# A chunked recurrence fused with two expert layers: the scores of both batch rows made where rows are turned, and their products in one run

## The chip, the cores and the metric

The kernel runs on one core of a Trainium2 chip. The metric is the device time of one execution in microseconds. The profile of the kernel before is one execution of it, with its own time.

## The reference, cut to what matters

Two batch rows of 768 positions, 8 heads of 48 columns. Three stages follow one another: a linear recurrence by heads, a dense layer pair with a normalization ahead of it, and a mixture of 8 experts in which each position goes to one.

```python
for t in range(S):                      # attention-like recurrence
    cur = np.einsum('bhd,bhe->bhde', u[None] * kt, vt)
    y[:, :, t] = np.einsum('bhd,bhde->bhe', rt, state + cur)
    state = w[None, :, :, None] * state + np.einsum('bhd,bhe->bhde', kt, vt)
x = y by position, 384 columns
xn = (x - mu) / np.sqrt(var + 1e-06) * g_ln
x = x + np.maximum(xn @ w_ch1, 0.0) @ w_ch2            # 384 -> 1536 -> 384
logits = x @ w_gate ; e = argmax, or the one before     # 8 experts, 384 -> 1024 -> 384
out[b, s] = p[e] * (np.maximum(x[b, s] @ w1[e], 0.0) @ w2[e])
```

## The kernel before

**Tiles.** The 1536 rows are 12 tiles of 128 positions, numbered c: tile c holds chunk c // 2 of batch row u = c % 2. Two tiles are a group, g = 0 to 5; I call g = 0 the first group, g = 1 the second, and so on. The recurrence is done by chunks. For each tile `scores` makes keys times queries inside the chunk (8 heads, two PSUM banks, halves of heads), VectorE multiplies them with a mask into `scT` (`masked`), `from_state` adds what the state carries in, `from_scores` what the masked scores give, both into one bank (this is the tile's product), and `gain` makes what the tile adds to the state. VectorE then does `new_state`, `sums` (product plus the diagonal part into `xs`) and `moments`; `rows_of` is the last two. The recurrence runs two tiles ahead of the dense layers: in group g the dense layers of tiles 2g, 2g + 1 are worked on, and the recurrence of tiles 2g + 2 and 2g + 3.

**The dense layers of a group.** `hidden(g, q)` makes pair q of six (q = 0 to 5): 18 matmuls of 256 columns into bank 6 or 7 by turns. ScalarE rectifies the pair into `hT_hi`, VectorE makes the remainder `hT_lo` (its `hidden`, line L1568) and counts `h_ready`. Two pairs later TensorE needs that bank again and waits for that count. `rows_out(g, u)` is the second layer, 36 matmuls into bank 5 - u; between its two calls `turn_xn(g + 1)` turns the normalized rows of the next group into banks 0 and 1. VectorE adds the result to the rows (`residual`), makes the turned rows' remainder (`turned`), and makes the gate columns of the expert layer (`gates`, L1677), nine for each tile, spread by hand between its other steps wherever nothing waits for them; a gate reads two tensors of SBUF, `x2` and `wgr`.

**What sets the order.** Every engine's program is written out by hand, with counting semaphores. In the kernel before, the loop body on TensorE is pairs 0 to 2, then `chunk` of the first tile (its gain and products), `scores` of the second tile, pairs 3 and 4, `chunk` of the second tile, pair 5, `rows_out`, `turn_xn`, `scores` of the next group's first tile in banks 2 and 3, and `rows_out`. GpSimd has a queue of its own order: `diagonal` of both tiles (after VectorE's `coefs`), then for each of the next two tiles `decays` (two products, L530 and L537, after the turned keys and queries of that tile have landed), `rows` (L548, L550) and `ends` (L563). SyncE's `load_turned(c)` waits until `from_state` of tile c - 2 is over, since it overwrites that tile's keys and queries.

```python
                for q in pairs:
                    if not isinstance(g, int) or g * NHP + q >= 2:
                        pe.wait_ge(h_ready, g * NHP + q - 1)
```

## Time and profile before

| what | us |
|---|---|
| median of 3 runs | 385.42 (384.82 to 387.62) |
| the profiled execution's own time | 384.97 |
| its span | 383.1 |
| mean granted TensorE clock | 0.996 |

The profiled execution took 1.9 us more than its span, and is 0.45 us below the median. The six groups fill the time from about 17 to 214 us of the span, the experts the rest.

### The profile page before, as it was taken

What the parts mean: (1) busy time and instruction counts of PE and PEld (TensorE: products, weight loads), DVE (VectorE), ACT (ScalarE), POOL (GpSimd) and SP (SyncE); (2) the same over time, 40 slices, a digit from 0 to 9 for tenths busy, and PEclk for the clock granted to TensorE, in tenths of its full rate; (3) what the DMA queues carried; (4) which work ended last, traced back from release to release, by engine and by line L of the source; (5) the groups of instructions that cost most, each with busy time, mean ns of one, the idle gap of its engine ahead of it and who ended that gap; (6) DMA issues with size and microseconds to landing.
All of it is one profiled execution on the core that took longest, in us unless ns stands there. A gap on an engine that the chain in (4) does not pass through costs nothing.

```text
span 383.1 us, 8871 instructions
## 1 busy us (share of the span) xinstructions
PE 372.5 (97%) x3056; PEld 338.6 (88%) x3056; DVE 285.5 (75%) x630; ACT 155.4 (41%) x281; POOL 137.5 (36%) x114
## 2 busy tenths in 40 slices
PE   8999999999999999999999999999999999999993
PEld 6899999999999999999999656789999999999982
DVE  7799899988897997868878568798546764647440
ACT  6556313212322221241441254368525852555530
POOL 2999784911760570100004006303332233223231
PEclk9999999999999999999999999999999999999998
DMA  7999603302500330500038484799874287111011
GB/s 218 328 329 285 212 22 113 112 21 67 157 36 21 110 110 26 181 3 22 21 97 286 134 308 144 264 372 305 301 277 151 87 277 284 43 34 43 26 45 43
DMA packets 32923, 56.67 MB, mean 148 GB/s; under 512 B 3294, under 2 KB 20484, under 8 KB 32753
## 3 DMA queue, kind: packets, MB, share of 16 engines
q1 hardware_dynamic: 30576, 49.84, 39.9%
q0 software_dynamic: 2304, 6.30, 5.3%
q8 instruction: 23, 0.38, 0.4%
q14 instruction: 20, 0.16, 0.1%
HBM read 51.41 MB, written 5.51 MB: 149 GB/s over the span
## 4 chain that ended last, share of the span: by engine, by line
PE 91%; DVE 5%; issue 1%; DMA 1%; ACT 1%; POOL 0%; SPq 0%; POOLq 0%; DVEq 0%; ACTq 0%
PE bank L1039 18%; PE bank L935 7%; PE bank L937 7%; PE bank L936 7%; PE bank L1367 5%; PE bank L1339 5%; PE bank L1375 5%; PE bank L1371 5%; PE bank L1343 5%; PE bank L1346 5%; PE bank L1356 3%; PE bank L953 3%; PE bank L1268 3%; PE bank L1245 3%; PE bank L984 2%; PE bank L974 2%
## 5 line engine op out<-in xcount | busy, mean ns | idle before, releaser
L1039 PE MATMUL bank<-xnT_hi,parts 128*128 128x256 f32 x432 | 65.3, 287 | 0.5 <-ACT xnT_hi L726 0.2
L1677 DVE SCALAR_TENSOR_TENSOR stage<-stage 128x384 f32<-128x384 f32 x81 | 60.7, 791 | 0.1
L1039 PEld LDWEIGHTS bank<-xnT_hi,parts 128*128 128x128 f32 x432 | 56.6, 191 | 2.0 <-ACT xnT_hi L726 0.5
L733 ACT ACTIVATE parts<-bank 128x512 fp32r<-128x512 f32 x36 | 21.5, 597 | 90.6 <-PE bank L1039 90.5
L667 POOL DMA_INDIRECT out_y<-late x14 | 20.5, 1462 | 93.9 <-DVE late L1964 93.9
L935 PE MATMUL bank<-parts 128*128 128x384 f32 x144 | 49.3, 342 | 0.0
L937 PE MATMUL bank<-parts 128*128 128x384 f32 x144 | 48.2, 335 | 0.0
L936 PE MATMUL bank<-parts 128*128 128x384 f32 x144 | 48.2, 334 | 0.0
L813 ACT ACTIVATE parts<-stage (+1 forms) x32 | 46.2, 1485 | 0.4 <-DMA stage<-in_w 0.4
L1933 DVE TENSOR_TENSOR parts<-stage,parts x24 | 41.1, 1755 | 4.9 <-ACT parts L813 4.2
L1039 PE MATMUL bank<-xnT_lo,parts 128*128 128x256 f32 x216 | 37.4, 282 | 0.0
L574 POOL TENSOR_TENSOR arena<-arena,coef 128x384 f32<-128x384 f32 x12 | 13.0, 1080 | 60.6 <-DVE coef L1458 60.3
L1568 DVE SCALAR_TENSOR_TENSOR parts<-bank,parts 128x512 fp32r<-128x512 f32 x36 | 24.8, 689 | 11.3 <-ACT parts L733 11.0
L1964 DVE TENSOR_SCALAR late<-bank,late 128x384 f32<-128x384 f32 x14 | 8.7, 618 | 32.9 <-PE bank L1375 32.6
L660 POOL DMA_INDIRECT late<-x_rows,late x18 | 22.3, 1241 | 28.2 <-DVE late L1890 23.0
L1039 PEld LDWEIGHTS bank<-xnT_lo,parts 128*128 128x128 f32 x216 | 30.9, 191 | 0.3 <-issue 0.3
L935 PEld LDWEIGHTS bank<-parts 128*128 128x128 f32 x144 | 27.1, 188 | 0.4
L936 PEld LDWEIGHTS bank<-parts 128*128 128x128 f32 x144 | 27.1, 188 | 0.0
L937 PEld LDWEIGHTS bank<-parts 128*128 128x128 f32 x144 | 27.0, 188 | 0.0
L1339 PE MATMUL bank<-parts,xnT_hi 128*128 (+1 forms) x84 | 26.6, 425 | 0.0
L904 ACT ACTIVATE heT_hi<-bank 128x512 fp32r<-128x512 f32 x28 | 15.2, 596 | 28.0 <-PE bank L1356 28.0
L1955 DVE TENSOR_TENSOR heT_lo<-bank,heT_hi 128x512 fp32r<-128x512 f32 x28 | 18.0, 683 | 11.0 <-ACT heT_hi L904 10.9
(257 smaller groups left out, 732.6 us busy)
## 6 DMA issues: line engine op xcount, KB each, us to landing
stage<-in_w SPq DMA_DIRECT2D x36, 768.0 KB, 6.7
stage<-in_w_ch SPq DMA_DIRECT2D x6, 768.0 KB, 7.8
arena<-in_k_t SPq DMA_DIRECT2D x12, 224.0 KB, 3.2
arena<-in_r_t SPq DMA_DIRECT2D x12, 224.0 KB, 3.1
arena<-in_v_rows SPq DMA_DIRECT2D x12, 192.0 KB, 3.9
arena<-in_k_rows SPq DMA_DIRECT2D x12, 192.0 KB, 3.2
x_rows<-stage SPq DMA_DIRECT2D x12, 192.0 KB, 1.9
arena<-in_r_rows SPq DMA_DIRECT2D x10, 192.0 KB, 3.3
```

The source lines that it names most:

```text
L660: pool.indirect_dma_start(xg[s % XR], None, x2_dram, bass.IndirectOffsetOnAxis(take[:, s:s + 1], 0)).then_inc(s_xg[s % XR], 16)
L667: pool.indirect_dma_start(out, bass.IndirectOffsetOnAxis(give[:, s:s + 1], 0), yo[s % 2], None, bounds_check=T - 1, oob_is_err=False).then ...
L733: act.activation(hT_hi[:, 2 * q:2 * q + 2, :].rearrange("p a t -> p (a t)"), bk[6 + q % 2][:], ACT.Relu).then_inc(h_hi_ready, 1)
L813: act.activation(e_at(b, 0, j), e_stage(h, j), ACT.Copy).then_inc(e_hi[j // EP], 1)
L935: pe.matmul(out_, a_lo, b_hi, start=start, stop=False)
L936: pe.matmul(out_, a_hi, b_lo, start=False, stop=False)
L937: return pe.matmul(out_, a_hi, b_hi, start=False, stop=stop)
L1039: mm = pe.matmul(acc, w[:, k, at], x[:, k, :], start=start and k == 0, stop=stop and k == KD - 1, skip_group_check=first and q == 0)
L1339: pe.matmul(bk[2 + half][:], xnT_hi[:, k, u], hi(k), start=k == 0, stop=False)
L1568: dve.scalar_tensor_tensor(hT_lo[:, at, :].rearrange("p a t -> p (a t)"), bk[6 + q % 2][:], 0.0, hT_hi[:, at, :].rearrange("p a t -> p (a ...
L1677: dve.scalar_tensor_tensor(spent[n % NSPENT], x2[t % 2], 1.0, wgr[e], ALU.mult, ALU.mult, accum_out=lg[:, t, e:e + 1]).then_inc(s_spent, 1)
L1933: dve.tensor_tensor(e_at(e & 1, 1, j), e_stage((e + 1) & 1, j), e_at(e & 1, 0, j).bitcast(F32), ALU.subtract).then_inc(e_lo[j // EP], 1)
```

## The change

**What it does.** From tile 4 on the scores of both tiles of the next group are made behind `turn_xn`, the first tile's in banks 6 and 7, the second's in banks 2 and 3. The masked scores of the two tiles go to two buffers, `scT[0]` and `scT[1]`. The products and gains of both tiles stand in one run behind pair 2, the first tile's in banks 4 and 3, the second's in banks 5 and 2. The second group makes its own scores behind its pair 0, in banks 0 to 3, and is now written out ahead of the loop, which runs over the third and the fourth group; the first group keeps its order, less the scores of tile 4 at its end. ScalarE scales both states (`decay`) in one place behind pair 1. VectorE masks the first tile's scores behind `turned`, makes both `coefs` behind pair 1, does both tiles' `new_state` and `rows_of` behind pair 2, and the gates are dealt out anew. SyncE's and GpSimd's programs are the same.

```diff
--- before.py
+++ after.py
@@ -753,13 +753,15 @@
                     round_piece(2)
                 hidden(g, range(1, 2))
                 decay(g * 2 + 2, 0)
+                if not first:
+                    decay(g * 2 + 3, 1)
                 hidden(g, range(2, 3))
...
-                decay(g * 2 + 3, 1)
+                    decay(3, 1)
@@ -940,11 +942,10 @@
                 if not isinstance(c, int) or c > 0:
                     pe.wait_ge(kdec_ready, c + 1)
                     pe.wait_ge(rdec_ready, c + 1)
-                if isinstance(c, int) and c < 4 and c >= 2 or u:
-                    if not isinstance(c, int) or c >= 2:
-                        pe.wait_ge(masked_ready, c * 2)
-                elif not isinstance(c, int) or c:
-                    pe.wait_ge(state_ready, c)
+                if isinstance(c, int) and 2 <= c <= 4:
+                    pe.wait_ge(masked_ready, c * 2)
+                elif u and not (isinstance(c, int) and c == 1):
+                    pe.wait_ge(state_ready, c - 1)
                 for p in range(NP_):
                     if isinstance(c, int) and c == 0:
                         pe.wait_ge(s_pair, p + 1)
@@ -1008,15 +1009,24 @@
                                        start=True, stop=True)
                 mm.then_inc(coef_mm, 1)
 
-            def chunk(c, u, n_lg, ends):
-                if ends:
-                    pe.wait_ge(state_ready, c)
-                    pe.wait_ge(masked_ready, c * 2 + 2)
-                    gain(c, u, bk[3])
-                if n_lg is not None:
-                    pe.wait_ge(x2_ready, n_lg)
-                from_state(c, u)
+            def first_chunk(c, u):
+                pe.wait_ge(state_ready, c)
+                gain(c, u, bk[3])
+                from_state(c, u, bk[4], c)
                 from_scores(c, u, bk[4], scT[0])
+
+            def chunks(g, ends):
+                c = g * 2 + 2
+                pe.wait_ge(masked_ready, c * 2 + 4)
+                pe.wait_ge(x2_ready, g * 2)
+                for u in range(2):
+                    if ends:
+                        pe.wait_ge(state_ready, c)
+                        gain(c + u, u, bk[3 - u])
+                    else:
+                        pe.wait_ge(s_rows[u], R_FIRST[u] + R_LOADS * (c // 2))
+                    from_state(c + u, u, bk[4 + u], c)
+                    from_scores(c + u, u, bk[4 + u], scT[u])
 
             def turn_xn(g):
                 for u in range(2):
@@ -1074,6 +1084,7 @@
             def rows_out(g, u, between=()):
                 if u == 0:
                     if not isinstance(g, int) or g >= 1:
+                        pe.wait_ge(x_ready, NT if isinstance(g, int) and g >= NG - 2 else g * 2 + 4)
                         pe.wait_ge(x2_ready, g * 2 - 1)
                 else:
                     pe.wait_ge(x_ready, NT if isinstance(g, int) and g >= NG - 2 else g * 2 + 4)
@@ -1125,32 +1136,34 @@
 
             def group(g, ends=True):
                 first = isinstance(g, int) and g == 0
-                n_lg = None if first else g * 2
 
                 pe.wait_ge(xnT_hi_ready, g * 2 + 2)
                 if first:
                     hidden(g, range(0, 2))
-                    scores(g * 2 + 2, 0, bk[0:2])
+                    scores(2, 0, bk[0:2])
                     hidden(g, range(2, 3))
-                    chunk(g * 2 + 2, 0, n_lg, ends)
+                    first_chunk(2, 0)
                     hidden(g, range(3, 5))
-                    scores(g * 2 + 3, 1, bk[0:2])
+                    scores(3, 1, bk[0:2])
                     hidden(g, range(5, NHP))
-                    chunk(g * 2 + 3, 1, n_lg, ends)
+                    first_chunk(3, 1)
                 else:
-                    hidden(g, range(0, 3))
-                    chunk(g * 2 + 2, 0, n_lg, ends)
-                    scores(g * 2 + 3, 1, bk[0:2])
-                    hidden(g, range(3, 5))
-                    chunk(g * 2 + 3, 1, n_lg, ends)
-                    hidden(g, range(5, NHP))
+                    if isinstance(g, int) and g == 1:
+                        hidden(g, range(0, 1))
+                        scores(4, 0, bk[0:2])
+                        scores(5, 1, bk[2:4])
+                        hidden(g, range(1, 3))
+                    else:
+                        pe.wait_ge(masked_ready, g * 4 + 6)
+                        hidden(g, range(0, 3))
+                    chunks(g, ends)
+                    hidden(g, range(3, NHP))
                 rows_out(g, 0)
                 turn_xn(g + 1)
                 if not first and ends:
-                    scores(g * 2 + 4, 0, bk[2:4])
+                    scores(g * 2 + 4, 0, bk[6:8])
+                    scores(g * 2 + 5, 1, bk[2:4])
                 rows_out(g, 1)
-                if first:
-                    scores(4, 0, bk[2:4])
 
             scores(0, 0, bk[0:2])
             pe.wait_ge(s_const, 16)
@@ -1175,7 +1188,8 @@
             keep_warm(1)
             group(0)
             pe.wait_ge(s_gw, 16)
-            with pe.Fori(1, NG - 2) as g:
+            group(1)
+            with pe.Fori(2, NG - 2) as g:
                 group(g)
             group(NG - 2, ends=False)
 
@@ -1461,8 +1475,8 @@
             def masked(c, banks, sc, halves=range(2)):
                 for half in halves:
                     dve.wait_ge(score_mm, c * 2 + half + 1)
-                    if not isinstance(c, int) or c >= 2:
-                        dve.wait_ge(y_mm, c)
+                    if c >= 2:
+                        dve.wait_ge(y_mm, c if c < 5 else c - 1)
                     dve.tensor_tensor(sc[:, NP_ * half:NP_ * (half + 1), :],
                                       banks[half][:].rearrange("p (a t) -> p a t", a=NP_),
                                       mask, ALU.mult).then_inc(masked_ready, 1)
@@ -1679,37 +1693,32 @@
 
             def group(g, ends=True):
                 t0, t1 = (g - 1) * 2, (g - 1) * 2 + 1
+                c0, c1 = g * 2 + 2, g * 2 + 3
                 if g > 1:
-                    gates(t0, range(4, 5))
+                    gates(t0, range(3, 5))
                 hidden(g, range(0, 1))
-                if not ends:
-                    coefs(g * 2 + 2, 0)
-                masked(g * 2 + 2, bk[2:4], scT[0])
-                gates(t0, range(5 if g > 1 else 4, 7))
+                if g == 1:
+                    masked(c0, bk[0:2], scT[0])
+                masked(c1, bk[2:4], scT[1])
+                if g > 1:
+                    gates(t0, range(5, 6))
                 hidden(g, range(1, 2))
-                if ends:
-                    coefs(g * 2 + 2, 0)
-                gates(t0, range(7, 8))
+                coefs(c0, 0)
+                coefs(c1, 1)
+                gates(t0, range(4 if g == 1 else 6, 7))
                 hidden(g, range(2, 3))
-                if ends:
-                    new_state(g * 2 + 2, 0, bk[3])
-                rows_of(g * 2 + 2, 0, bk[4])
-                if not ends:
-                    coefs(g * 2 + 3, 1)
-                masked(g * 2 + 3, bk[0:2], scT[0])
-                if ends:
-                    coefs(g * 2 + 3, 1)
-                gates(t0, range(8, E + 1))
+                for c, u in ((c0, 0), (c1, 1)):
+                    if ends:
+                        new_state(c, u, bk[3 - u])
+                    rows_of(c, u, bk[4 + u])
+                gates(t0, range(7, E + 1))
                 hidden(g, range(3, 4))
-                gates(t1, range(0, 1))
+                gates(t1, range(0, 2))
                 hidden(g, range(4, 5))
-                if ends:
-                    new_state(g * 2 + 3, 1, bk[3])
-                rows_of(g * 2 + 3, 1, bk[4])
                 means(g + 1)
-                gates(t1, range(1, 2))
+                gates(t1, range(2, 4))
                 hidden(g, range(5, NHP))
-                gates(t1, range(2, E + 1))
+                gates(t1, range(4, E + 1))
                 rows_done(g)
 
             def rows_done(g):
@@ -1718,8 +1727,10 @@
                     flags(0)
                 residual(g, 0)
                 turned(g + 1)
+                if 0 < g < NG - 2:
+                    masked(g * 2 + 4, bk[6:8], scT[0])
                 if g < NG - 2:
-                    gates(g * 2, range(0, 4))
+                    gates(g * 2, range(0, 3 if g else 4))
                 elif g == NG - 2:
                     gates(g * 2, range(0, 6))
                 residual(g, 1)
```

On TensorE, in the body of the loop before (second to fourth group), from the first tile's gain (L965) to pair 3; the REGISTER_ALU rows make the semaphores' targets:

```order
L965 MATMUL bank<-arena 48x48 x8
L970 REGISTER_ALU
L974 MATMUL bank<-arena 64x96 x8
L980 REGISTER_ALU
L984 MATMUL bank<-arena 64x48 x16
L941 REGISTER_ALU
L945 REGISTER_ALU
L953 MATMUL bank<-arena 128x128 x8
L1045 REGISTER_ALU
L1039 MATMUL bank<-xnT_hi,parts 128x256 x6
```

In the changed kernel the same place, in the second group, which is written out (the loop has the same order); L1049 is the pairs' matmul, L966 the gain, L975 and L985 the products:

```order
L1049 MATMUL bank<-xnT_lo,parts 128x256 x3
L966 MATMUL bank<-arena 48x48 x8
L975 MATMUL bank<-arena 64x96 x8
L985 MATMUL bank<-arena 64x48 x16
L966 MATMUL bank<-arena 48x48 x8
L975 MATMUL bank<-arena 64x96 x8
L985 MATMUL bank<-arena 64x48 x16
L1049 MATMUL bank<-xnT_hi,parts 128x256 x6
```

The second tile's gain and product now follow the first tile's at once, and the scores (L953 there) are gone from the place.

On VectorE, in the third group of the kernel before, from the gate ahead of pair 2 to pair 3 (L1677 gate, L1568 pair, L1481 and L1482 new state, L1488 and L1496 `rows_of`, L1466 masks, L1458 coefs):

```order
L1677 SCALAR_TENSOR_TENSOR stage,lg<-stage 128x384
L1568 SCALAR_TENSOR_TENSOR parts<-bank,parts 128x512
L1481 TENSOR_TENSOR arena<-bank,arena 48x4x48
L1482 TENSOR_TENSOR arena<-bank,arena 48x4x48
L1488 TENSOR_TENSOR stage<-bank,arena 128x384
L1496 BN_STATS stats<-stage 128x6
L1466 TENSOR_TENSOR arena<-bank,cst 128x512 x2
L1458 TENSOR_REDUCE coef<-arena 128x8
L1677 SCALAR_TENSOR_TENSOR stage,lg<-stage 128x384
L1568 SCALAR_TENSOR_TENSOR parts<-bank,parts 128x512
```

In the changed kernel, same group and same two pairs (L1691 gate, L1582 pair, L1495 and L1496 new state, L1502 and L1510 `rows_of`):

```order
L1691 SCALAR_TENSOR_TENSOR stage,lg<-stage 128x384
L1582 SCALAR_TENSOR_TENSOR parts<-bank,parts 128x512
L1495 TENSOR_TENSOR arena<-bank,arena 48x4x48
L1496 TENSOR_TENSOR arena<-bank,arena 48x4x48
L1502 TENSOR_TENSOR stage<-bank,arena 128x384
L1510 BN_STATS stats<-stage 128x6
L1495 TENSOR_TENSOR arena<-bank,arena 48x4x48
L1496 TENSOR_TENSOR arena<-bank,arena 48x4x48
L1502 TENSOR_TENSOR stage<-bank,arena 128x384
L1510 BN_STATS stats<-stage 128x6
L1691 SCALAR_TENSOR_TENSOR stage,lg<-stage 128x384 x2
L1582 SCALAR_TENSOR_TENSOR parts<-bank,parts 128x512
```

Masks and coefs have left the stretch between the two pairs; the second tile's new state and rows, and one more gate, have come into it.

## Rows read from the trace of the kernel before

**Rows 1.** The page: busy share of TensorE, and the chain by engine.

```profile
PE 372.5 (97%) x3056; PEld 338.6 (88%) x3056; DVE 285.5 (75%) x630; ACT 155.4 (41%) x281; POOL 137.5 (36%) x114
...
PE 91%; DVE 5%; issue 1%; DMA 1%; ACT 1%; POOL 0%; SPq 0%; POOLq 0%; DVEq 0%; ACTq 0%
```

**Rows 2.** Windows, third and fifth group: sum, PE, PEld, DVE, ACT, POOL, clock, DMA.

```profile
85.19:118.21 33.02, 33.02 (x347) 32.20 (x347) 28.50 (x71) 8.74 (x24) 14.60 (x12) 1.00 0.25 75
...
151.23:182.24 31.01, 31.01 (x299) 30.40 (x299) 24.81 (x81) 8.74 (x24) 1.67 (x2) 1.00 0.20 65
```

**Rows 3.** Timeline of TensorE, third group: start, us, line, operation.

```profile
90.58 0.88 PE L1039 MATMUL bank<-xnT_hi,parts 128*128 128x256 f32 x6
91.30 0.52 PE L1039 MATMUL bank<-xnT_lo,parts 128*128 128x256 f32 x3
91.75 0.56 PE L965 MATMUL bank<-arena 128*48 128x48 f32 x16
...
92.82 1.09 PE L984 MATMUL bank<-arena 128*64 128x48 f32 x32
93.84 1.16 PE L953 MATMUL bank<-arena 48*128 48x128 f32 x16
94.93 0.97 PE L1039 MATMUL bank<-xnT_hi,parts 128*128 128x256 f32 x6
95.74 0.52 PE L1039 MATMUL bank<-xnT_lo,parts 128*128 128x256 f32 x3
...
110.75 1.16 PE L953 MATMUL bank<-arena 48*128 48x128 f32 x16
```

**Rows 4.** Timeline of VectorE, same stretch.

```profile
90.93 0.69 DVE L1568 SCALAR_TENSOR_TENSOR parts<-bank,parts 128x512 fp32r<-128x512 f32 x1
91.53 0.54 DVE L1458 TENSOR_REDUCE coef<-arena 128x8 f32<-128x384 f32 x1
91.99 0.55 DVE L1677 SCALAR_TENSOR_TENSOR stage<-stage 128x384 f32<-128x384 f32 x1
...
92.49 0.69 DVE L1568 SCALAR_TENSOR_TENSOR parts<-bank,parts 128x512 fp32r<-128x512 f32 x1
...
93.96 0.56 DVE L1488 TENSOR_TENSOR stage<-bank,arena 128x384 f32<-128x384 f32 x1
...
95.03 1.29 DVE L1466 TENSOR_TENSOR arena<-bank,cst 128x512 f32<-128x512 f32 x2
...
98.61 1.00 DVE L1677 SCALAR_TENSOR_TENSOR stage<-stage 128x384 f32<-128x384 f32 x1
```

**Rows 5.** Timeline of ScalarE, same stretch.

```profile
90.19 1.17 ACT L686 ACTIVATE arena<-arena,w_chunk 112x96 f32<-112x96 f32 x4
```

**Rows 6.** Timeline of GpSimd, third group; in brackets the idle time before, and releaser.

```profile
92.15 1.08 POOL L574 TENSOR_TENSOR arena<-arena,coef 128x384 f32<-128x384 f32 x1 [14.26 <-DVE coef L1458]
...
97.90 1.30 POOL L530 TENSOR_TENSOR arena<-arena 112x512 f32<-112x512 f32 x1
99.15 1.59 POOL L537 TENSOR_TENSOR arena<-arena 112x512 f32<-112x512 f32 x1
...
104.59 1.30 POOL L530 TENSOR_TENSOR arena<-arena 112x512 f32<-112x512 f32 x1 [0.82 <-DMA arena<-in_k_t]
```

**Rows 7.** Timeline of SyncE's queue, third group: first load of each tile.

```profile
93.20 0.36 SPq L406 DMA_DIRECT2D arena<-in_r_t  x1
...
100.86 0.34 SPq L406 DMA_DIRECT2D arena<-in_r_t  x1
```

**Rows 8.** Timeline of VectorE, second group.

```profile
55.23 0.69 DVE L1568 SCALAR_TENSOR_TENSOR parts<-bank,parts 128x512 fp32r<-128x512 f32 x1
...
65.59 2.61 DVE L1677 SCALAR_TENSOR_TENSOR stage<-stage 128x384 f32<-128x384 f32 x1
```

**Rows 9.** Timeline of TensorE at the second group's start.

```profile
50.97 1.16 PE L953 MATMUL bank<-arena 48*128 48x128 f32 x16
```

**Rows 10.** Timeline of GpSimd, the sixth tile's turned keys.

```profile
51.51 1.60 POOL L537 TENSOR_TENSOR arena<-arena 112x512 f32<-112x512 f32 x1
```

More of the change, by code:

```diff
@@ L967, in gain, with from_state @@
                 mm.then_inc(gain_mm, 1)
-            def from_state(c, u):
+            def from_state(c, u, bank, before):
                 pe.wait_ge(state_ready, c - 1)
-                pe.wait_ge(x_ready, c)
+                pe.wait_ge(x_ready, before)
                 for p in range(NP_):
                     for rows in HALVES:
-                        mm = pe.matmul(bk[4][rows, p * PD:(p + 1) * PD], rT[u][:, p, rows], state[u][:, p, :],
+                        mm = pe.matmul(bank[rows, p * PD:(p + 1) * PD], rT[u][:, p, rows], state[u][:, p, :],
                                        start=p == 0, stop=False, skip_group_check=True)
```

## The prediction

> **What bounds the kernel now.** I read the page first: TensorE is busy 97% of the span, and 91% of the chain that ended last lies on it [rows 1]. The windows by group then say whether anything is to be had inside a group: in the third group TensorE is busy in 33.02 of 33.02 us at full clock [rows 2]. No wait is left there to remove. A group gets shorter only by what is lost between kinds of matmul, and longer as soon as TensorE has to wait. So two things are to be costed: changes of kind on TensorE, and whether each thing that TensorE asks for is still there in time when VectorE's steps are dealt out anew.
>
> **What the run saves.** In the third group six matmuls of a pair start 0.72 us before the next three (90.58 to 91.30), so three take 0.36; but from the last three of pair 2 to the gain it is 0.45, and the first six of pair 3 take 0.81 (94.93 to 95.74) [rows 3]. Leaving the pairs' full-array matmuls for the small ones, and coming back, costs 0.09 us each way, 0.18 together. Before, a group leaves three times (first tile, second tile, behind `turn_xn`); after it, twice. The same holds for the second group, where the scores of tile 4 left their place between two groups and stand behind pair 0, but one run less is made behind pair 2; and for the fifth, where only the two products are joined. Four groups, 4 x 0.18 = 0.7 us. The number of matmuls stays the same. Inside the runs a change from product to scores goes too (92.82 to 93.84 for the second part of a product, 1.02 us ahead of the scores [rows 3]); if it hides another 0.09 us, 4 x 0.27 = 1.1 us. Nothing shows it apart, so I take 0.7 and keep 1.1 as the bound.
>
> The Trainium skill, "TensorEngine Tiling (Array Packing)", Key Properties, says that a change of tiling mode drains the engine; the 0.09 us agree, and product to scores would be such a change (other row and column tiles), which is the 1.1.
>
> **What it asks of the others.** Pair 5 needs the bank of pair 3, so TensorE may start it only when VectorE has done pair 3. Before, the second chunk stood between pairs 4 and 5 on TensorE, and the second tile's new state and rows behind pair 4 on VectorE; now both come ahead of pair 3. I follow the third group, in the times of the trace of before (its start is the same row).
>
> TensorE: the run starts at 91.75. First tile: gain and state part to 92.82, product to 93.84, 2.09 us; second tile the same, to 95.93. Pair 3 is 0.09 and 2 x (0.72 + 0.36) = 2.16 us, to 98.18, pair 4 to 100.34 [rows 3]. There pair 5 asks for pair 3.
>
> VectorE: pair 1 comes at 90.93 before; the same steps stand ahead of it, less one gate of 0.5 us, so 90.45 [rows 4]. Pair 0.60, two coefs of 0.46: 91.97 [rows 4]. Then gate 6. GpSimd's diagonal product starts 0.62 us after coefs start [rows 4, 6], here at 91.67, for 1.0 us, and the gate meets it. What such a meeting costs: the gate at 91.99, ahead of GpSimd's 92.15, took 0.5 us, the one at 98.61, into a GpSimd product that ran from 97.90 to 99.15, took 1.00 and ended 0.4 us after that product did [rows 4, 6]. Gate 6 ends at 92.7 + 0.4 = 93.1. ScalarE's two scalings (from 90.19, 1.17 each [rows 5]) put pair 2's data at about 93.0, so this costs nothing yet. From pair 2 to `sums` 1.47 us, `sums` and moments 1.07, new state 1.47 - 0.60 = 0.87, `sums` and moments again 1.07 [rows 4]: 93.1 + 4.48 = 97.58. Then gates 7 and 8.
>
> GpSimd: `from_state` of the first tile ends at 92.82 and SyncE issues the loads 0.38 us later, at 93.20, as before [rows 3, 7]. From this issue to the first product it is 3.73 us where GpSimd waits for the data (100.86 to 104.59 [rows 6, 7]). Before, GpSimd still had the second diagonal to do and began at 97.90; now it is free and begins at 96.93. Two products of 1.25 and 1.56 us [rows 6] end at 98.18 and 99.74. Both gates fall into them: gate 7 ends at 98.18 + 0.4 = 98.6, gate 8 at 99.74 + 0.4 = 100.15. Pair 3 on VectorE ends at 100.15 + 0.69 = 100.84 [rows 4], and TensorE has been waiting since 100.34: **0.5 us**, and the same in the fourth group.
>
> Second group: TensorE starts pair 0 at 50.87, 0.10 ahead of the scores of before [rows 9]. Pair 0 to 53.03, two tiles' scores (0.09, 2 x 1.09 [rows 3]) to 55.30, pairs 1 and 2 with the way back to 59.71, the run from 59.80 to 63.98, pairs 3 and 4 to 68.39. VectorE is late here: pair 0 at 55.23 [rows 8], two tiles' masks (four of 0.6) and pair 1 to 58.95, coefs to 59.87, then three gates beside the two diagonals of about 1.1 us each, to 62.8; 4.48 more, 67.28. GpSimd begins at 59.80 + 1.07 + 0.38 + 3.73 = 64.98; its second product ends at 67.5, the third at 68.7, the gates at 67.9 and 69.1, pair 3 at 69.8. TensorE waits **1.4 us** from 68.39. Behind the gates stand pair 3 and, through pair 5, all of `rows_out`.
>
> Fifth group: no decays are left, GpSimd is busy 1.67 us in all [rows 2], and there is no new state. Gates take 0.5 us, pair 3 is done about 1 us before it is asked for. No wait.
>
> Other new waits, at nothing: the scores of tile 5 need GpSimd's keys by 54.2, they are ready at 53.1 [rows 10], 1.1 us of cover; behind `turn_xn` scores stood at 110.75 in the third group [rows 3], the second tile's now come about 111.8, and GpSimd, from 96.93 with two decays, three products and two decays more of 1.0 to 1.6 us each [rows 6], has that tile's keys by 107 at the latest; the masks of banks 6 and 7, for which the next group's first pair waits, have from there to 118.2 [rows 2], over 6 us, for 1.2 us of masks and the two turning steps ahead of them. SyncE's second load starts some 5 us earlier, which only keeps GpSimd busy without a break. Were the 1.1 us of cover gone, each us over would be a us of time.
>
> **The sum.** 1.4 + 0.5 + 0.5 - 0.7 = +1.7 us on the profiled execution's 384.97, 386.7. That execution lies 0.4 below the median; I name **387.0**. What is next late after pair 3: pair 5's remainder, asked for 5.2 us into `rows_out`, has about 0.7 us left where four gates meet GpSimd ahead of it.
>
> A rule on the meeting: the Trainium skill, "SBUF — State Buffer", "SBUF: two separate sides", has VectorE (with two SBUF inputs) and GpSimd share ports under an exclusive lock, held for the whole instruction by whoever started first. By that each gate costs at most one product of GpSimd. The gate at 65.59 took 2.61 us and so sat through two [rows 8], so the trace has a longer price also.
>
> **Rivals.**
> *The gates miss GpSimd.* If new state and rows are over sooner, or the data lands later than 3.73 us after the issue, gates 7 and 8 take 0.48 each and end at 98.5; pair 3's data is there at 99.0 and VectorE is done at 99.7, 0.6 us before TensorE asks. Only the second group keeps a wait of some 0.6 us or none. Against it: GpSimd is 0.6 us into its product when the gates begin, by the numbers above. Time 384.97 - 0.7 to -0.1, at the median 384.7 to 385.3; with 1.1 saved and no wait 384.3. This is the side where the change gains, by under 0.3%.
>
> *Gates sit through two products.* One gate of 2.61 us instead of 1.3 between `rows_of` and pair 3 puts 1.3 us on the wait of its group. It decides from its first 0.1 us, since VectorE is already behind; one in each of three groups would be 3 x 1.3 = 3.9 on top, 391, slower by 1.4%. One such gate in all: 388.3. For it is that VectorE now meets GpSimd with nine gates or so between pairs 2 and 5 instead of three, with GpSimd busy without a break; against it that most gates that meet it, as at 98.61, wait for one.
>
> *The change doesn't save a change of kind.* If product to gain of the second tile costs as much as the way back did, the 0.7 is 0.35, and the time 387.3.
>
> **Chances.** Waits at pair 3 of 1 to 3.5 us in all, as worked out: 0.55. Gates miss, small gain or nothing: 0.28. Two-product gates or a second wait at pair 5's remainder, 388.5 and more: 0.14. Anything else, a late load or a loop entry: 0.03. The range goes from 384.2 (gain with 1.1 saved) to 389.4 (two gates that sit through two products). A measurement of this kernel can tell about 1% from no change: faster by that (under 381.6) has no mechanism, 0.01; slower (over 389.3) 0.07; within 0.92.
>
> **What would show it.** Right: in the timeline of TensorE the last pair of a group starts late by 1.4 us in the second group and 0.5 in the third and fourth, the wait put down to VectorE's pair line; gates ahead of pair 3 of 1.0 us and more; first decays of GpSimd 1 us earlier than before relative to the group; 0.09 us lost on four transitions of a group and not six. Wrong: TensorE without a break, groups of 32.84 us; then the step on the gates' meeting has failed. It would be wrong by more if TensorE waited at the scores of tile 5 or at a group's start for the masks.

## The result, and the profile after

| | before | changed |
|---|---|---|
| median of 13 runs each, us | 386.21 (384.32 to 387.62) | 389.43 (384.61 to 390.94) |
| profiled execution, us | 384.97 | 389.43 |
| its span, us | 383.1 | 387.6 |

The ratio is 1.0068 (95% interval 1.0046 to 1.009): the change costs 2.6 us by the ratio, 3.2 by the medians, and its executions lie 6 us apart where those of before lie 3 us apart. All ratios here leave out executions more than 1.5% above the fastest of their own kernel: the two longest of the change, and further down the four longest of the kernel with later loads and the longest of the kernel with the long wait. The profiled execution of the change is 4.5 us above that of before. It is its kernel's median, while that of before lies 1.2 us below its own, so the two traces differ by more than the kernels do.

The page of the changed kernel, the rows that answer to [rows 1] and the group of the pairs' matmuls:

```profile
PE 372.8 (96%) x3056; PEld 339.5 (88%) x3056; DVE 288.3 (74%) x630; ACT 155.0 (40%) x281; POOL 140.0 (36%) x114
...
PE 72%; DVE 14%; issue 4%; DMA 3%; POOL 3%; SPq 1%; ACT 1%; DVEq 0%; POOLq 0%
...
L1049 PE MATMUL bank<-xnT_hi,parts 128*128 128x256 f32 x432 | 65.8, 289 | 3.6 <-DVE parts L1582 3.3
```

TensorE has the same work and is no longer without a break: the chain now lies on it for 72% of the span, not 91%, and 14% on VectorE. The matmuls of the pairs have 3.6 us of idle time ahead of them, 3.3 of it put down to VectorE's pair line, where they had 0.5 in all. By group (answers to [rows 2]; the second group first, which now makes the scores of four tiles: its own two behind pair 0, and the next group's two behind `turn_xn`):

```profile
51.15:90.12 38.97, 36.75 (x379) 35.55 (x379) 34.96 (x77) 8.63 (x24) 20.90 (x17) 0.96 0.22 66
90.12:123.56 33.44, 32.79 (x348) 32.08 (x347) 30.72 (x71) 8.70 (x24) 15.21 (x12) 1.00 0.25 76
123.56:156.75 33.19, 32.78 (x348) 32.07 (x348) 28.72 (x71) 8.63 (x24) 12.83 (x10) 1.00 0.25 75
```

The third group took 33.02 us before and takes 33.44, of which TensorE is busy 32.79. The fourth takes 33.19, with 32.78 busy. The sums: from the second group's start to the end of the fifth group it was 131.28 us (50.97 to 182.25), and is 135.22 (51.15 to 186.37), 3.94 more; the rest of the 4.5 us lies outside these groups. TensorE, third group, from the end of pair 2 to pair 5 (answers to [rows 3], columns as there):

```profile
96.68 0.56 PE L966 MATMUL bank<-arena 128*48 128x48 f32 x16
...
97.75 1.09 PE L985 MATMUL bank<-arena 128*64 128x48 f32 x32
98.67 0.53 PE L966 MATMUL bank<-arena 128*48 128x48 f32 x16
...
99.71 1.09 PE L985 MATMUL bank<-arena 128*64 128x48 f32 x32
100.73 0.98 PE L1049 MATMUL bank<-xnT_hi,parts 128*128 128x256 f32 x6
...
104.78 0.52 PE L1049 MATMUL bank<-xnT_lo,parts 128*128 128x256 f32 x3
105.96 0.98 PE L1049 MATMUL bank<-xnT_hi,parts 128*128 128x256 f32 x6 [0.65 <-DVE parts L1582]
```

The first tile's product and the second's gain are 0.92 us apart (97.75 to 98.67), the second's product and pair 3 1.02 (99.71 to 100.73): the end of the small matmuls costs 0.1 us when the kind changes. The last three matmuls of pair 4 start at 104.78, pair 5 should come at 105.14 and comes at 105.96. VectorE in the same stretch (answers to [rows 4]):

```profile
101.62 0.56 DVE L1510 BATCH_NORM_STATS2 stats<-stage 128x6 f32<-128x384 f32 x1
102.10 1.62 DVE L1691 SCALAR_TENSOR_TENSOR stage<-stage 128x384 f32<-128x384 f32 x1
...
103.65 1.64 DVE L1691 SCALAR_TENSOR_TENSOR stage<-stage 128x384 f32<-128x384 f32 x1
...
105.22 0.68 DVE L1582 SCALAR_TENSOR_TENSOR parts<-bank,parts 128x512 fp32r<-128x512 f32 x1
```

and GpSimd (answers to [rows 6]):

```profile
102.01 1.29 POOL L530 TENSOR_TENSOR arena<-arena 112x512 f32<-112x512 f32 x1 [3.47 <-DMA arena<-in_k_t]
103.26 1.61 POOL L537 TENSOR_TENSOR arena<-arena 112x512 f32<-112x512 f32 x1
```

and ScalarE, which rectifies pair 3:

```profile
103.19 0.60 ACT L733 ACTIVATE parts<-bank 128x512 fp32r<-128x512 f32 x1 [5.35 <-PE bank L1049]
```

Here is the whole loss of a group in a few rows. The new state and rows of both tiles are done at 102.10. GpSimd has begun its decays at 102.01, so the first gate sits until GpSimd's product is over at 103.26 and takes 1.55 us to the next step, the second sits through the next product, until 105.22; only then comes pair 3 (L1582), and TensorE starts 0.74 us after its start. Pair 3's data came out of ScalarE at about 103.8 (103.19 and 0.60), so the first gate delayed nothing; the second made pair 3 late. In the second group the wait on TensorE is longer:

```profile
68.27 0.52 PE L1049 MATMUL bank<-xnT_lo,parts 128*128 128x256 f32 x3
71.00 0.98 PE L1049 MATMUL bank<-xnT_hi,parts 128*128 128x256 f32 x6 [2.22 <-DVE parts L1582]
71.82 0.55 PE L1049 MATMUL bank<-xnT_lo,parts 128*128 128x256 f32 x3
72.18 1.47 PE L1049 MATMUL bank<-xnT_hi,parts 128*128 128x256 f32 x6
73.44 0.84 PE L1049 MATMUL bank<-xnT_lo,parts 128*128 128x256 f32 x3
```

Pair 5 was due at 68.63 and comes 2.37 us later. (The 2.22 in brackets, here and elsewhere, is the idle time alone, which starts at the modelled end of the matmuls before.) VectorE and GpSimd ahead of it:

```profile
49.20 1.12 DVE L1691 SCALAR_TENSOR_TENSOR stage<-stage 128x384 f32<-128x384 f32 x1 [1.96 <-DMA stage<-in_gate_rows]
...
68.23 0.54 DVE L1691 SCALAR_TENSOR_TENSOR stage<-stage 128x384 f32<-128x384 f32 x1
...
68.70 1.64 DVE L1691 SCALAR_TENSOR_TENSOR stage<-stage 128x384 f32<-128x384 f32 x1
...
70.27 0.68 DVE L1582 SCALAR_TENSOR_TENSOR parts<-bank,parts 128x512 fp32r<-128x512 f32 x1
```

```profile
68.21 1.68 POOL L537 TENSOR_TENSOR arena<-arena 112x512 f32<-112x512 f32 x1
```

Here only the second of the two gates is long, beside the product from 68.21. The first took 0.54 us, although it started 0.02 us behind that product. The wait is longer because VectorE came late: both tiles' rows were done at 68.23, 0.4 us before TensorE asked for pair 3. One reason is the first row above: the first of all gates waited 1.96 us for the landing of the weights of the ninth gate column (the ninth row, below).

The matmuls behind the wait are slow from 72.2 on (1.26 us for six that take 0.72). The windows of that stretch (clock is the third value from the end):

```profile
71.00:72.00 1.00, 1.00 (x8) 1.00 (x9) 1.00 (x3) 0.00 (x0) 0.92 (x2) 1.00 0.02 8
72.00:73.00 1.00, 1.00 (x7) 1.00 (x7) 1.00 (x3) 0.00 (x0) 1.00 (x2) 0.59 0.00 0
73.00:75.00 2.00, 2.00 (x10) 2.00 (x9) 2.00 (x6) 0.68 (x2) 2.00 (x2) 0.50 0.00 0
75.00:76.00 1.00, 1.00 (x6) 1.00 (x5) 1.00 (x3) 1.00 (x3) 1.00 (x2) 0.70 0.09 16
76.00:77.00 1.00, 1.00 (x7) 1.00 (x7) 1.00 (x2) 0.30 (x2) 1.00 (x2) 1.00 0.02 8
```

TensorE had been idle for 2.22 us up to 71.0. Some 1.2 us after it started again the granted clock fell to half, the lower of its two levels, and it came back at about 75.5. Pair 5 and the 36 matmuls of the first `rows_out` took 3.08 and 6.95 us, not 2.25 and 6.25 as in the third group: 1.5 us lost to the clock.

The sum of the loss: 2.37 + 0.82 + 0.57 of waits for pair 3, 0.14 ahead of pair 2 in the second group, and 1.5 of clock, 5.4 us together. The groups are only 3.9 us longer, so the new order saves 1.5 us on TensorE over the four groups.

### The profile page after: what moved, and what is told of

Same layout as the page of the kernel before. It is cut to its first block, busy times and chain, and to the rows that moved or that the text cites. A ratio compares the mean times of both kernels' runs of the same rounds, so it can differ in the third digit from the quotient of the medians.

```text
span 387.6 us, 8854 instructions
## 1 busy us (share of the span) xinstructions
PE 372.8 (96%) x3056; PEld 339.5 (88%) x3056; DVE 288.3 (74%) x630; ACT 155.0 (40%) x281; POOL 140.0 (36%) x114
## 4 chain that ended last, share of the span: by engine, by line
PE 72%; DVE 14%; issue 4%; DMA 3%; POOL 3%; SPq 1%; ACT 1%; DVEq 0%; POOLq 0%
PE bank L1049 9%; PE bank L937 6%; PE bank L939 5%; PE bank L938 5%; PE bank L1381 5%; PE bank L1353 5%; PE bank L1389 5%; PE bank L1385 5%; PE bank L1357 5%; PE bank L1360 5%; DVE stage L1691 4%; PE bank L1370 3%; PE bank L1282 3%; PE bank L1259 3%; PE bank L954 2%
## 5 line engine op out<-in xcount | busy, mean ns | idle before, releaser
L1049 PE MATMUL bank<-xnT_hi,parts 128*128 128x256 f32 x432 | 65.8, 289 | 3.6 <-DVE parts L1582 3.3
L1691 DVE SCALAR_TENSOR_TENSOR stage<-stage 128x384 f32<-128x384 f32 x81 | 65.8, 855 | 2.1 <-DMA stage<-in_gate_rows 2.0
L1049 PEld LDWEIGHTS bank<-xnT_hi,parts 128*128 128x128 f32 x432 | 57.2, 193 | 5.6 <-DVE parts L1582 4.4
L1049 PE MATMUL bank<-xnT_lo,parts 128*128 128x256 f32 x216 | 37.7, 284 | 0.0
L574 POOL TENSOR_TENSOR arena<-arena,coef 128x384 f32<-128x384 f32 x12 | 14.1, 1192 | 51.8 <-DVE coef L1472 51.4
L1049 PEld LDWEIGHTS bank<-xnT_lo,parts 128*128 128x128 f32 x216 | 31.3, 193 | 0.0
L1582 DVE SCALAR_TENSOR_TENSOR parts<-bank,parts 128x512 fp32r<-128x512 f32 x36 | 24.7, 687 | 5.6 <-ACT parts L733 5.4
```

The source lines that it names most:

```text
L1049: mm = pe.matmul(acc, w[:, k, at], x[:, k, :], start=start and k == 0, stop=stop and k == KD - 1, skip_group_check=first and q == 0)
L1582: dve.scalar_tensor_tensor(hT_lo[:, at, :].rearrange("p a t -> p (a t)"), bk[6 + q % 2][:], 0.0, hT_hi[:, at, :].rearrange("p a t -> p (a ...
L1691: dve.scalar_tensor_tensor(spent[n % NSPENT], x2[t % 2], 1.0, wgr[e], ALU.mult, ALU.mult, accum_out=lg[:, t, e:e + 1]).then_inc(s_spent, 1)
```

## Experiments

Each is compared with the kernel before on the same chip; times are medians of 4 to 12 runs. The chips differ between experiments, and before's median goes from 385.61 to 385.77, so two experiments are best compared by their ratios. Waits and single rows are of one profiled execution each.

**Two gates behind pair 3.**

```diff
-                gates(t0, range(7, E + 1))
                 hidden(g, range(3, 4))
+                gates(t0, range(7, E + 1))
                 gates(t1, range(0, 2))
```

> The changed kernel with two gates of each group (columns 7 and 8 of the first tile) moved from ahead of pair 3 to behind it on VectorE; all else as changed. Theory A, the two gates that meet GpSimd make TensorE wait for pair 3: its wait ahead of the last pair (2.4, 0.8 and 0.6 us in the second, third and fourth group) falls to nothing in the third and fourth group and below 1.2 us in the second. The gates are then in the way of pair 5's remainder, for which I expect a new wait of 0.5 to 1.5 us near the end of the first rows_out of a group. Time 1 to 3 us below the changed kernel, about that of before. Theory B, the second tile's new state and rows ahead of pair 3 are too much by themselves: pair 3 is late by 0.4 us or more in the third and fourth group even so, and the time stays within 1 us of the changed kernel.

385.5 us against 385.75 of before, ratio 1.0003 (0.9982 to 1.0023). That is 3.9 us below the changed kernel's median, 2.5 by the ratios. No wait is left ahead of the last pair. The new one is where it was expected, ahead of the last sixth of the first `rows_out`, but smaller: the third and fourth group take 32.79 and 32.76 us, some 0.3 above those of the next kernel, which has none; the second 35.17, 0.5 above. So the place of two gates is the whole loss against before (1.0068 against 1.0003), and the new state and rows alone are not too much (theory B falls).

**Gates spread.**

```diff
-                gates(t0, range(4 if g == 1 else 6, 7))
+                gates(t0, range(4 if g == 1 else 6, 6 if g == 1 else 7))
...
-                gates(t0, range(7, E + 1))
                 hidden(g, range(3, 4))
-                gates(t1, range(0, 2))
+                gates(t0, range(6 if g == 1 else 7, E + 1))
                 hidden(g, range(4, 5))
+                gates(t1, range(0, 1 if g == 1 else 2))
                 means(g + 1)
-                gates(t1, range(2, 4))
                 hidden(g, range(5, NHP))
-                gates(t1, range(4, E + 1))
+                gates(t1, range(1 if g == 1 else 2, E + 1))
```

> The changed kernel with the gates dealt out so that none stands between the products' rows and pair 3, at most two between pairs 4 and 5, and the others behind pair 5, where VectorE had time left until rows_out ends. Theory A (VectorE lateness through gates that meet GpSimd is the whole loss): TensorE has no idle time in the third and fourth group, which take 32.6 us, and under 0.5 us in the second, where the granted clock stays at its higher level; time 1.2 to 1.8 us below before, ratio 0.996. Theory B (something of the run itself costs, the banks, the loads or the loop): third and fourth group take 33.0 us or more without a wait for pair 3, and the time is that of before or above.

383.85 us (382.5 to 384.18), ratio 0.9934 (0.9911 to 0.9957): 2.5 us below before by the ratio, more than the 1.2 to 1.8 expected, and 1.9 by the medians. VectorE, third group:

```profile
97.15 0.56 DVE L1510 BATCH_NORM_STATS2 stats<-stage 128x6 f32<-128x384 f32 x1
99.34 0.69 DVE L1582 SCALAR_TENSOR_TENSOR parts<-bank,parts 128x512 fp32r<-128x512 f32 x1 [1.63 <-ACT parts L733]
99.95 0.55 DVE L1691 SCALAR_TENSOR_TENSOR stage<-stage 128x384 f32<-128x384 f32 x1
...
100.43 1.36 DVE L1691 SCALAR_TENSOR_TENSOR stage<-stage 128x384 f32<-128x384 f32 x1
```

After the second tile's rows (97.15) VectorE has nothing to do for 1.63 us and waits for pair 3's data; the gate behind it that meets GpSimd (1.36 us) has no one waiting.

**Loads later.** Nothing on VectorE or TensorE is changed; GpSimd only begins later.

```diff
-                    sp.wait_ge(state_mm, c - 3)
+                    sp.wait_ge(state_mm, c - 3 if u or isinstance(c, int) else c - 2)
```

> The changed kernel, where the loads of the first tile's keys and queries wait for the second tile's state product, not the first's, so that GpSimd begins its decays some 2 us later; VectorE's order as changed. Theory A, GpSimd's products make the gates ahead of pair 3 long: in the third and fourth group both gates take 0.55 us and TensorE waits for nothing at the last pair; in the second group VectorE is later and still meets GpSimd, a wait of 1 us or more stays. Time 1 to 1.6 us below the changed kernel. Theory B, it is the number of VectorE's steps: waits of 0.8 and 0.6 us stay in the third and fourth group, whatever GpSimd does, and the time is that of the changed kernel or higher.

385.5 us in the median, ratio 0.9976 (0.9951 to 1.0), but in two heaps: seven of twelve runs from 382.36 to 385.75, one at 387.66, four from 389.68 to 390.04. The profiled execution (382.36) in the third group, VectorE:

```profile
97.87 0.54 DVE L1691 SCALAR_TENSOR_TENSOR stage<-stage 128x384 f32<-128x384 f32 x1
...
98.33 0.55 DVE L1691 SCALAR_TENSOR_TENSOR stage<-stage 128x384 f32<-128x384 f32 x1
...
99.58 0.69 DVE L1582 SCALAR_TENSOR_TENSOR parts<-bank,parts 128x512 fp32r<-128x512 f32 x1 [0.69 <-ACT parts L733]
```

and GpSimd:

```profile
100.22 1.68 POOL L530 TENSOR_TENSOR arena<-arena 112x512 f32<-112x512 f32 x1 [5.91 <-DMA arena<-in_k_t]
```

GpSimd begins at 100.22, both gates take 0.5 us, and TensorE waits for nothing. With the same steps in the same order on VectorE, the meeting with GpSimd alone decides: theory B falls. The wait of 1 us or more that I expected to stay in the second group was not there either: GpSimd began at 67.38 in it, the second gate at 67.08, and both gates took 0.5 us. So that group missed GpSimd by a few tenths of a us. There is no trace of the second heap; it needed another run (below).

**Two runs.** The second tile's run goes back behind pair 4.

```diff
                 for u in range(2):
+                    if u:
+                        hidden(g, range(3, 5))
...
-                    hidden(g, range(3, NHP))
+                    hidden(g, range(5, NHP))
```

(On VectorE the second tile's new state and rows stand behind pair 4 again.)

> The changed kernel with the one run undone: the second tile's gain and products stand behind pair 4 again, its new state and rows behind pair 4 on VectorE; scores, banks and buffers as changed. Theory A, the run's place makes VectorE late: no wait ahead of pair 5 in the third and fourth group. What is saved there against before is then only what scores in one place save. If leaving and coming back costs 0.18 us only, as I took it, a group takes 33.0 us; if the small matmuls' own ends hold another 0.1 us at each change of kind, as the groups of the changed kernel less their waits suggest (32.6 us with the run), it takes 32.9 us with two runs. Time 0.3 to 0.8 us below before. Theory B: the wait for pair 3 stays, time as the changed kernel.

386.92 us, ratio 1.003 (1.0003 to 1.0057), no better than before: a miss. No wait stood ahead of the last pair, as theory A said, but another had taken its place, in a row that I had not thought of:

```profile
73.33 0.44 PE L937 MATMUL bank<-parts 128*128 128x384 f32 x1 [1.66 <-DVE stage L1504]
```

The second tile's product now lies in bank 5, which the first `rows_out` writes, so that one waits for the second tile's rows (L1504 is `sums` here). In the change the run's early place hides this. The ninth row landed late here too (first gate at 48.59). It was no clean measurement of the run, so I made it again with both products in bank 4 and without the wait that the change put ahead of the first `rows_out`:

> Two runs again (the second tile's gain and product behind pair 4), now with both products in bank 4, so that the first rows_out of a group, which writes bank 5, no longer waits for the second tile's rows; scores in one place as in the change. It measures what the one run alone saves on TensorE. Expected: no wait over 0.3 us in the third and fourth group; a group takes 32.8 us (the spread kernel's 32.53 and 0.28 for one more leaving and return), if a return costs 0.19 with the end of the small matmuls; 32.7 if it costs 0.09 as I took it. Time about 1 us above the spread kernel and 1 us below before.

385.45 us, ratio 0.9997 (0.9976 to 1.0018). The fourth group, free of waits, took 32.83 us (119.29 to 152.12), the third 33.44. Its extra 0.6 us lies ahead of the last sixth of the first `rows_out`, which waited for pair 5's remainder; I had expected at most 0.3. The 32.83 for a group, against 32.52 with one run, bears out about 0.3 us for leaving and coming back. I expected about 1 us below before, and the time is that of before; the waits that stayed are part of it.

**A long wait in the second group.** The spread kernel, with one wait more ahead of the second group's last pair:

```diff
-                    hidden(g, range(3, NHP))
+                    hidden(g, range(3, 5))
+                    if isinstance(g, int) and g == 1:
+                        pe.wait_ge(h_ready, g * NHP + 5)
+                    hidden(g, range(5, NHP))
```

> The kernel with the gates spread, in which TensorE in the second group alone waits ahead of its last pair for pair 4's remainder, which VectorE makes some 3.8 us after TensorE comes there; nothing else is changed. Theory A, a wait of over 2 us costs more than itself, since the granted clock falls behind it as it did in the changed kernel (0.5 to 0.6 for 3 us behind a wait of 2.4): TensorE idle 3.5 to 4 us, granted clock about half for 2 to 4 us afterwards, time 5 to 6 us above the kernel with the gates spread. Theory B, the fall of the clock in the changed kernel had nothing to do with the wait: clock stays at 1.0 and the time is 3.8 us above.

388.47 us (385.9 to 392.43), ratio 1.0052 (1.0025 to 1.008), so 4.6 us above the spread kernel by the medians and 4.5 by the ratios. The profiled execution was the longest one; its wait was 5.2 us, more than the 3.8 intended:

```profile
69.90:75.16 5.26, 0.05 (x2) 0.01 (x1) 5.26 (x8) 0.60 (x1) 5.18 (x5) 0.72 0.36 110
75.16:77.00 1.84, 1.84 (x8) 1.84 (x9) 1.04 (x4) 0.00 (x0) 1.84 (x2) 0.50 0.00 0
77.00:79.00 2.00, 2.00 (x12) 2.00 (x11) 0.00 (x0) 0.00 (x0) 1.92 (x3) 0.50 0.00 0
79.00:81.00 2.00, 2.00 (x13) 2.00 (x13) 1.05 (x2) 1.68 (x4) 1.20 (x2) 0.99 0.03 8
```

The granted clock is at 0.50 from the first matmul for almost 4 us. This group took 41.91 us, 7.2 more than the spread kernel's 34.70, so some 1.9 beyond the wait (theory A). That the lower clock followed this wait is shown by the one trace; how much a wait of a given length costs beyond itself is not, since the four runs differ by 6.5 us.

**The ninth row.** In the profiled execution of the change the first gates began at 49.20, behind the landing of the ninth gate column's weights. In the kernels with two gates moved, gates spread and later loads they began at about 47.2, in the first kernel with two runs at 48.59. I took that wait to the ninth column, in the changed kernel, the spread kernel, the kernel with later loads and the kernel before:

```diff
                     dve.wait_ge(s_gr, 16)
-                    dve.wait_ge(s_g9, 16)
                 for e in columns:
+                    if t == 0 and e == E:
+                        dve.wait_ge(s_g9, 16)
```

> The changed kernel, where VectorE waits for the ninth gate column's row of weights only at the ninth column, not ahead of the first gate. Theory A, the late landing of that row (gates began at 49.2 in the profiled execution of the change, at 47.2 in those of its variants) makes VectorE late in the second group and is what spreads the changed kernel's times from 384.6 to 390.9: first gate at 47.3 or sooner in each execution, the second group's wait 1.3 us or less, median 386 to 387.5 and all runs within 3 us. Theory B, the spread comes from elsewhere (which of GpSimd's products a gate meets): median and spread as the changed kernel's, 389 and 6 us.

387.42 us (385.17 to 389.01), ratio 1.0043 (1.0018 to 1.0068). That is 2.0 us below the change by the medians but 1.0 by the ratios, whose intervals overlap, and six runs spread over 3.8 us in place of thirteen over 6.3. So what the row costs is not clear of the noise, and that it spreads the times is likely and not shown. The first gates began at 47.0, and TensorE was still idle for 1.81 us in the second group, over the 1.3 that I gave:

```profile
70.06 0.98 PE L1049 MATMUL bank<-xnT_hi,parts 128*128 128x256 f32 x6 [1.81 <-DVE parts L1582]
```

The granted clock fell to 0.50 behind this wait as well. Theory A is half right at most: a wait of almost 2 us for TensorE, and the lower clock, are there without the late row.

> The kernel with the gates spread and the ninth row waited for only at the ninth column. If VectorE has time enough once the gates are spread, the late row costs nothing there: time equal to the spread kernel's 383.9 within 0.5 us, no idle time of TensorE in the second to fourth group. If the second group is still near its limit, 0.5 to 1 us below it and a narrower spread.

382.24 us (382.0 to 383.54), ratio 0.9922 (0.9906 to 0.9939): 3.0 us below before, the lowest median of the study. It is 1.6 us below the spread kernel by the medians, but only 0.5 by the ratios, and the intervals overlap: between the two the runs don't decide. Its groups have no idle time on TensorE:

```profile
50.94:85.55 34.61, 34.61 (x380) 33.85 (x379) 33.55 (x72) 8.74 (x24) 19.97 (x17) 1.00 0.24 74
85.55:118.07 32.52, 32.52 (x347) 32.01 (x347) 29.05 (x73) 8.74 (x24) 15.11 (x12) 1.00 0.27 78
118.07:150.60 32.53, 32.53 (x348) 32.02 (x347) 27.54 (x71) 8.74 (x24) 12.29 (x10) 1.00 0.26 77
```

> The changed kernel with its order of VectorE untouched, the first tile's loads 2 us later and the ninth gate row waited for only at the ninth column. The kernel with later loads alone had times in two heaps, 382.4 to 385.8 and 387.7 to 390.0. Theory A, the second heap is executions in which the ninth row lands late, VectorE is about 2 us later in the second group and its gates meet GpSimd after all: now one heap, 382.3 to 386, median 383.5 to 384.5, ratio to before 0.995. Theory B, the heaps come from GpSimd or TensorE alone: both heaps stay.

384.47 us (383.69 to 385.96), ratio 0.9968 (0.9951 to 0.9984), twelve runs in one heap. The second heap of the kernel with later loads (five of twelve) is gone, as theory A says, so the late row is what made it, as far as twelve runs each on two chips can show. The profiled execution still has a wait of 1.12 us in the second group, where one gate met GpSimd; the clock stayed at 1.00 behind it.

> The kernel before with the ninth gate row waited for only at the ninth column, nothing else. In the kernel before TensorE waits for nothing in the second group even when VectorE is late there by 2 us, if my reading holds that its pairs 3 and 5 lie further apart: time as before within 0.3%, ratio 0.999 to 1.001. If the late row costs the kernel before as well, the ratio is 0.995 to 0.998, and part of what the spread kernel gained is not the change's.

385.82 us against 385.77, ratio 0.9996 (0.9981 to 1.001). The kernel before doesn't care when that row lands. So what the spread kernels gain comes from the change with its gates in new places, not from the row.

## Why the prediction was right, and where its terms were off

**Direction and mechanism: right.** The predicted chain stands in the trace of the third and fourth group step by step. Both gates ahead of pair 3 met GpSimd's decays, in the third group for 1.55 and 1.57 us. Pair 3 was late, and TensorE waited ahead of the last pair in the second, third and fourth group and not in the fifth. In the second group one of the two gates met GpSimd, where I had both. Moving the two gates, or moving GpSimd away from them, took the waits away; the other reading, too many steps on VectorE, doesn't explain that.

**The number: too low, and near by luck.** I named 387.0, 1.6 us above the median of before that I had, 385.42. The runs give 2.6 us by the ratio, which is 388.0 from the same start. The changed kernel's median itself, 389.43, is at the very upper end of my range (389.4), against a before of 386.21 this time. My sum gave +1.7 on the profiled execution; these groups grew by 3.94. The waits were 1.4 us too small and another wait of 0.14 was missing, the clock's 1.5 was missing, and the saving was 0.8 too small: the last error hid part of the others. Two roundings don't matter to this: 386.7 and the 0.45 below the median are 387.15, and two gates through two products would be 387.0 + 2.6 = 389.6.

**Size of the waits: too small.** I had 1.4 + 0.5 + 0.5 = 2.4 us, and the profiled execution has 2.37 + 0.82 + 0.57 = 3.76. In the third group the steps stand close to where I put them. Counted from the group's start (85.19 in my sum, 90.12 in the trace), both tiles' rows are done at 11.98 us, where I had 12.39, but that lead is worth nothing, since the gates wait for GpSimd: it begins at 11.89 (I had 11.74), its two products take 1.25 and 1.61 us (1.25 and 1.56), the second gate ends at 15.10 (14.96), and TensorE starts at 15.84 (15.65), having asked at 15.02 instead of 15.15. Small errors of 0.19 and 0.13 us on both sides of a short wait make 0.5 into 0.82; the wait is the difference of two sums of fifteen us and was never known better than that. In the second group it is 2.37 for 1.4. There the late row moved VectorE's pair 0 to 57.03, 5.88 us behind the group's start, where I had 4.36 (50.87 to 55.23). I had no term for it: in the trace of before the row's landing delayed nothing. But it explains only part. In the changed kernel without that wait, pair 0 stood 4.37 us behind the group's start (50.90 to 55.27), as I had it, and pair 5, due at 68.09, still came 1.97 us late, at 70.06. So by these two executions 0.40 us is the row's, and about 0.57 is left for my chain: TensorE asked 0.33 us sooner than I had it (17.19 us behind the start, not 17.52), and started 0.23 us later (19.16, not 18.93).

**The clock: missing.** A wait of 2.4 us was followed by matmuls at half clock that cost 1.5 us more. I added waits to busy time as if the rate stayed. The trace of before has full clock in all these groups, so nothing in it priced this; it belonged into the range as an unknown that only adds.

**What the run saves: too small.** I took 0.18 us for a group, 0.7 in all, and 1.1 as the bound. The groups without a wait take 32.52 us, 0.50 less than before; over the four groups of the changed kernel, 1.5 us. Two rows tell where it was missed. Product to gain of the second tile takes 0.92 us where product to scores took 1.02, and two tiles' scores in a row take 1.99 (two of 1.09 before), so at each end of a kind of small matmuls 0.1 us lies in the row of the block that ends, ahead of the 0.09 that I saw on the next. Leaving and coming back then costs 0.28 us, which the two-run kernel's 32.83 against 32.52, 0.31 apart, bears out. The Trainium skill, "TensorEngine Tiling (Array Packing)", Key Properties, says that a change of tiling mode drains the engine, without a price. The rows agree in kind, with 0.09 to 0.19 us at a change, and the 1.1 that I had kept as the bound for it was too low.

**Rivals.** "The gates miss GpSimd" is what the kernel with later loads shows: time below before. I gave it 384.3 to 385.3, and the seven shorter runs, 382.4 to 385.8, reach lower still, since the run saves more than I had. "Gates sit through two products" didn't come true on the critical gates; what made the time exceed my number was the clock, the late row and waits longer than worked out. The other waits that I put at nothing (GpSimd's keys for tile 5, masks ahead of a group, scores of the second tile) were nothing. The next late thing that I named, pair 5's remainder, came up as soon as the two gates were moved behind pair 3.

The surplus of 4.5 us between the two profiled executions is not the typical one: by the medians it is 3.2 us and by the ratio 2.6. The execution of before lay 1.2 us below its median, and that of the change on its own.

## What to carry to other kernels

When work is gathered on the bound engine, each step that another engine must do for it moves ahead too: ask which count the bound engine waits for two or three steps later, and keep fill-in work behind that step, not ahead of it. Fill-in instructions have the price of their place: the gates here, which read two SBUF tensors, took 0.5 us beside an idle GpSimd, mostly 0.9 to 1.6 beside a busy one, and 2.6 at worst, so deal them out by what GpSimd does then. A wait on a load that is only needed eight steps later cost nothing in the kernel before, where there was slack; where there was none it came with 1.0 to 2.0 us in the medians, a cost that the ratios leave open. Put such a wait at the first step that needs the load.

## What the runs showed of the hardware that I had not expected

The granted clock of TensorE fell to half behind idle times of 1.81, 2.22 and 5.21 us in otherwise full work, for 3 to 4 us (0.50 in the windows from 73 to 75 us and from 75.2 to 79), and stayed at 1.00 behind idle times of 0.65, 1.12 and 1.66 us, the last one in the first kernel with two runs. Each is a single trace. The end of a block of small matmuls costs 0.1 us inside the block's own row when the kind changes next, and nothing when the same kind goes on.
